# One 256-column operand for the high and low parts of the rows in tiles of 128 rows

## What is computed

```python
def _moe_ref(x, w_gate, w_noise, noise, w1, w2):     # D=192, E=8, F=1024
    ...
    for e in range(E):
        for k in range(2):
            mask = top2[:, k] == e
            ...
            h = np.maximum(x[mask] @ w1[e], 0.0)
            out[mask] += top2_w[mask, k, None] * (h @ w2[e])
def _moe2_ref(x, w_gate, w1, w2):
    ...
        xe = x[mask]
        h = np.maximum(xe @ w1[e], 0.0)
        ye = h @ w2[e]
        out[mask] = gate_w[mask, None] * ye
```

## Time and profile before

| | us |
|---|---|
| median of 3 runs | 1208.05 (1206.38 to 1210.27) |
| the profiled execution | 1204.87 |
| its span, first to last instruction | 1203.1 |
| PE busy | 1090.5 (91%) |
| DVE busy | 793.1 (66%) |
| ACT busy | 591.3 (49%) |
| POOL busy | 526.6 (44%) |

### The profile page before, as it was taken

How to read it: one execution, slowest core, us unless ns; L and a number is a source line. 1 busy time by engine, 2 the same in 40 slices (tenths; PEclk the granted TensorE clock), 3 DMA queues, 4 the chain that set the end, 5 groups by cost and what they waited for, 6 DMA issues and landing times.

```text
span 1203.1 us, 28405 instructions
## 1 busy us (share of the span) xinstructions
PE 1090.5 (91%) x8218; PEld 1053.8 (88%) x8219; DVE 793.1 (66%) x1352; ACT 591.3 (49%) x1082; POOL 526.6 (44%) x621
## 2 busy tenths in 40 slices
PE   3962999999999999999999999999999888999995
PEld 1541989999999999999999999988999888999995
DVE  9998889996787554555595545545655964655652
ACT  2340555665654555667535445445754434444442
POOL 1000456665444544443455544444443434545552
PEclk9985899999999999999999999999998989999998
DMA  7152223324522326421327233266432473543510
GB/s 248 53 164 74 67 63 89 84 80 145 147 87 83 110 76 211 148 88 63 86 78 220 90 89 107 77 201 181 123 103 66 138 215 104 143 121 105 143 42 22
DMA packets 97780, 136.47 MB, mean 113 GB/s; under 512 B 25994, under 2 KB 75981, under 8 KB 97484
## 3 DMA queue, kind: packets, MB, share of 16 engines
q1 hardware_dynamic: 78284, 92.96, 26.0%
q0 software_dynamic: 19456, 43.04, 12.3%
HBM read 104.74 MB, written 34.54 MB: 116 GB/s over the span
## 4 chain that ended last, share of the span: by engine, by line
PE 62%; DVE 17%; issue 8%; DMA 7%; ACT 2%; DVEq 1%; POOL 1%; ACTq 0%; POOLq 0%; SPq 0%; PEldq 0%
PE ps_y L1492 18%; PE ps_y L1493 8%; PE ps_h L1462 6%; PE ps_h L1472 6%; PE ps_h L1466 6%; PE ps_h L1463 6%; PE ps_h L1469 6%; DMA row<-x_rows,read_now 5%; DVE prod L592 4%; DVE h_lo L923 2%; PE ps_x L1448 2%; PE ps_x L1449 1%; DVE prod L604 1%; DVE prod L809 1%; PE ps_route L1396 1%
## 5 line engine op out<-in xcount | busy, mean ns | idle before, releaser
L1492 PE MATMUL ps_y<-w_hl,h_hi 128*128 128x384 f32 x1480 | 451.8, 369 | 15.8 <-DVE h_lo L923 15.2
L923 DVE SCALAR_TENSOR_TENSOR h_lo<-ps_h,h_hi 128x512 fp32r<-128x512 f32 x404 | 258.9, 685 | 241.0 <-ACT h_hi L1238 205.2
L1493 PE MATMUL ps_y<-w_hl,h_lo 128*128 128x192 f32 x1480 | 373.6, 252 | 0.0
L1238 ACT ACTIVATE h_hi<-ps_h 128x512 fp32r<-128x512 f32 x404 | 219.4, 595 | 220.3 <-PE ps_h L1472 209.1
L1492 PEld LDWEIGHTS ps_y<-w_hl,h_hi 128*128 128x128 f32 x1480 | 282.1, 191 | 21.5 <-DVE h_lo L923 20.3
L1493 PEld LDWEIGHTS ps_y<-w_hl,h_lo 128*128 128x128 f32 x1480 | 286.5, 194 | 0.0
L488 POOL DMA_INDIRECT row<-x_rows,read_now x202 | 229.5, 1136 | 119.6 <-POOL read_now L484 81.9
L1462 PE MATMUL ps_h<-xa_hi,w1a_hi 128*128 128x256 f32 (+1 forms) x808 | 234.8, 291 | 8.4 <-issue 5.3
L1466 PE MATMUL ps_h<-xa_lo,w1a_hi 128*128 128x256 f32 (+1 forms) x808 | 230.1, 285 | 2.1 <-DVE xa_lo L912 2.1
L1472 PE MATMUL ps_h<-xb_lo,w1b_hl 128*128 128x256 f32 (+1 forms) x808 | 229.8, 284 | 0.0
L1463 PE MATMUL ps_h<-xa_hi,w1a_lo 128*128 128x256 f32 (+1 forms) x808 | 229.2, 284 | 0.0
(11 more groups left out here) (184 smaller groups left out, 1328.3 us busy)
## 6 DMA issues: line engine op xcount, KB each, us to landing
w_raw<-in_moe_w_dram SPq DMA_DIRECT2D x32, 768.0 KB
w1a_raw<-in_moe_w_dram SPq DMA_DIRECT2D x32, 512.0 KB
w1b_raw<-in_moe_w_dram SPq DMA_DIRECT2D x64, 256.0 KB
x_pad<-in_x_dram SPq DMA_DIRECT2D x2, 2688.0 KB, 10.4
x_pad<-y_rows SPq DMA_DIRECT2D x14, 384.0 KB
prod<-y_rows SPq DMA_DIRECT2D x14, 384.0 KB
x_rows<-tok SPq DMA_DIRECT2D x4, 1344.0 KB
row<-x_rows,read_now POOLq DMA_INDIRECT x202
```

Of the source, the lines that this page charges most:

```text
L923: nc.vector.scalar_tensor_tensor(out=h_lo[:, i * GF:(i + 1) * GF, :], in0=ps_h[:, i, :].rearrange("p (f t) -> p f t", f=GF), scalar=0.0, i ...
L1238: act.activation(h_hi[:, i * GF:(i + 1) * GF, :], ps_h[:, i, :].rearrange("p (f t) -> p f t", f=GF), ACT.Relu).then_inc(h_hi_ready, 1)
L1492: nc.tensor.matmul(ps_y[:, u, 0:2 * D], h_hi[:, i, cols], w2_hl[b][:, f, :], start=(i == 0), stop=False)
L1493: last = nc.tensor.matmul(ps_y[:, u, 0:D], h_lo[:, i, cols], w2_hl[b][:, f, 0:D], start=False, stop=(i == FC - 1))
```

## The change

The high and the low part of a row tile now stand side by side in one buffer (`xa[:, 0]` and `xa[:, 1]`, the same for `xb`). Tiles of 256 rows compute as before. A half tile takes another way on three engines.

- PE (`up_half`): w1a_hi meets the high and low parts in one matmul of 256 columns, w1b_hl the same, and w1a_lo meets xa_hi in 128. The first block has four matmuls, the other seven have three: 25 in place of 40. What belongs to the high parts lands in one half of a block of ps_h, what belongs to the low parts in the other. The groups become ready one by one.
- ACT copies the second halves of a group out of ps_h (`copy_part`, 256 columns). DVE adds the first halves (`sum_parts`, 256 columns). ACT rectifies the sum to h_hi (`high_of_sum`), and DVE makes h_lo of it (`low_of_sum`). ACT's order is copy 0, copy 1, high 0, the side work, copy 2, high 1, copy 3, high 2, high 3; DVE's is its side work, sum 0, sum 1, low 0, sum 2, low 1, sum 3, low 2, low 3.
- ACT and DVE choose the way with a branch in every tile. DVE's registers for the next expert are loaded in `next_expert`, ahead of the groups, instead of behind them.

```diff
-        xa_hi = sb("xa_hi", [P, T], F32R)
-        xa_lo = sb("xa_lo", [P, T], F32R)
-        xb_hh = sb("xb_hh", [P, T], F32R)
-        xb_lo = sb("xb_lo", [P, T], F32R)
+        xa = sb("xa", [P, 2, T], F32R)
+        xb = sb("xb", [P, 2, T], F32R)
+        xa_hi, xa_lo = (xa[:, i, :] for i in range(2))
+        xb_hh, xb_lo = (xb[:, i, :] for i in range(2))
         h_hi = sb("h_hi", [P, FC, T], F32R)
         h_lo = sb("h_lo", [P, FC, T], F32R)
+        sum_more = sb("sum_more", [P, T])
...
+        h_part = tok_T[:, 1, :].rearrange("p (i f t) -> p i f t", i=2, t=P)
+        h_sum = [buf.rearrange("p (f t) -> p f t", t=P) for buf in (tok_T_b[:, 1, :], sum_more[:, :])]
...
+        def half_parts(i):
+
+            return [ps_h[:, i, :].rearrange("p (f v t) -> p v f t", f=GF, v=2)[:, v, :, :] for v in range(2)]
...
+            def next_expert(p, j):
+
+                with dve.If(dve.snap(expert_at) == j):
...
+                    dve.reg_load(expert_at, table[p][0:1, bass.ds(e * 4 + 1, 1)])
+                    dve.reg_load(half_at, table[p][0:1, bass.ds(e * 4 + 2, 1)])
+                    dve.reg_mov(split_1a_at, j)
+                    dve.reg_sub(split_1b_at, expert_at, 1)
...
+            def split_w1_ahead(p, j):
+
+                with dve.If(dve.snap(split_1a_at) == j):
+                    split_w1a(*ahead())
...
+            def sum_parts(g0, j, i):
+
+                dve.wait_ge(h_part_copied, (g0 + j) * NG + (i + 1))
+                if i > 1:
+                    dve.wait_ge(h_lo_ready, (g0 + j) * NG + (i - 1))
+                nc.vector.tensor_tensor(h_sum[i % 2], half_parts(i)[0], h_part[:, i % 2, :, :],
+                                        ALU.add).then_inc(h_summed, 1)
+
+            def low_of_sum(g0, j, i):
+
+                dve.wait_ge(h_hi_ready, (g0 + j) * NG + (i + 1))
+                nc.vector.scalar_tensor_tensor(
+                    out=h_lo[:, i * GF:(i + 1) * GF, 0:P], in0=h_sum[i % 2], scalar=0.0,
+                    in1=h_hi[:, i * GF:(i + 1) * GF, 0:P].bitcast(F32), op0=ALU.max, op1=ALU.subtract).then_inc(h_lo_ready, 1)
...
-                for i in range(NG):
-                    dve.wait_ge(h_hi_ready, (g0 + j) * NG + (i + 1))
-                    nc.vector.scalar_tensor_tensor(
-                        out=h_lo[:, i * GF:(i + 1) * GF, :], in0=ps_h[:, i, :].rearrange("p (f t) -> p f t", f=GF),
-                        scalar=0.0, in1=h_hi[:, i * GF:(i + 1) * GF, :].bitcast(F32), op0=ALU.max, op1=ALU.subtract).then_inc(h_lo_ready, 1)
+                if weights:
+                    next_expert(p, j)
+                with dve.If(dve.snap(half_at) == j):
+                    for i in range(NG):
+                        sum_parts(g0, j, i)
+                        if i > 0:
+                            low_of_sum(g0, j, i - 1)
+                    low_of_sum(g0, j, NG - 1)
+                with dve.Else():
+                    for i in range(NG):
+                        dve.wait_ge(h_hi_ready, (g0 + j) * NG + (i + 1))
+                        nc.vector.scalar_tensor_tensor(
+                            out=h_lo[:, i * GF:(i + 1) * GF, :], in0=ps_h[:, i, :].rearrange("p (f t) -> p f t", f=GF),
+                            scalar=0.0, in1=h_hi[:, i * GF:(i + 1) * GF, :].bitcast(F32), op0=ALU.max, op1=ALU.subtract).then_inc(h_lo_ready, 1)
+                    dve.sem_inc(h_summed, NG)
...
-            def tile(p, g0, n, b0, j, ahead):
-
-                for i in range(NG):
-                    act.wait_ge(h_ps, (g0 + j) * NG + (i + 1))
-                    act.activation(h_hi[:, i * GF:(i + 1) * GF, :], ps_h[:, i, :].rearrange("p (f t) -> p f t", f=GF),
-                                   ACT.Relu).then_inc(h_hi_ready, 1)
-                    if i == NG // 2 - 1:
-                        side_early(p, j)
-                        if ahead is not None:
-                            with act.If(j == b0):
-                                split_w1a(*ahead)
-                        side_late(p, j)
-                        act.sem_inc(ps_x_free, 1)
+            def mid_tile(p, j, b0, ahead):
+
+                side_early(p, j)
+                if ahead is not None:
+                    with act.If(j == b0):
+                        split_w1a(*ahead)
+                side_late(p, j)
+                act.sem_inc(ps_x_free, 1)
+
+            def copy_part(g0, j, i):
+
+                act.wait_ge(h_ps, (g0 + j) * NG + (i + 1))
+                act.activation(h_part[:, i % 2, :, :], half_parts(i)[1], ACT.Copy).then_inc(h_part_copied, 1)
+
+            def high_of_sum(g0, j, i):
+
+                act.wait_ge(h_summed, (g0 + j) * NG + (i + 1))
+                act.activation(h_hi[:, i * GF:(i + 1) * GF, 0:P], h_sum[i % 2], ACT.Relu).then_inc(h_hi_ready, 1)
+
+            def copy_high(g0, j, i):
+
+                act.wait_ge(h_ps, (g0 + j) * NG + (i + 1))
+                act.activation(h_hi[:, i * GF:(i + 1) * GF, :], ps_h[:, i, :].rearrange("p (f t) -> p f t", f=GF),
+                               ACT.Relu).then_inc(h_hi_ready, 1)
+
+            def tile(p, g0, n, b0, full, j, ahead):
+
+                with act.If(j < full):
+                    for i in range(NG // 2):
+                        copy_high(g0, j, i)
+                with act.Else():
+                    for i in range(NG // 2):
+                        copy_part(g0, j, i)
+                    high_of_sum(g0, j, 0)
+                mid_tile(p, j, b0, ahead)
+                with act.If(j < full):
+                    for i in range(NG // 2, NG):
+                        copy_high(g0, j, i)
+                    act.sem_inc(h_part_copied, NG)
+                with act.Else():
+                    for i in range(NG // 2, NG):
+                        copy_part(g0, j, i)
+                        high_of_sum(g0, j, i - 1)
+                    high_of_sum(g0, j, NG - 1)
...
+            def up_half(p, g0, j, b):
+
+                for f in range(FC):
+                    cols = slice(f * P, (f + 1) * P)
+                    at = f % GF * T
+                    dst = ps_h[:, f // GF, at:at + T]
+                    if f == 0:
+                        nc.tensor.matmul(dst[:, 0:P], w1a_hi[b][:, cols], xa[:, 0, 0:P], start=True, stop=False)
+                        nc.tensor.matmul(dst[:, 0:P], w1a_lo[b][:, cols], xa[:, 0, 0:P], start=False, stop=False)
+                        pe.wait_ge(x_lo_ready, 2 * (g0 + j) + 1)
+                        nc.tensor.matmul(dst[:, P:T], w1a_hi[b][:, cols], xa[:, 1, 0:P], start=False, stop=False)
+                        pe.wait_ge(x_hi_ready, 2 * (g0 + j) + 2)
+                        pe.wait_ge(x_lo_ready, 2 * (g0 + j) + 2)
+                    else:
+                        nc.tensor.matmul(dst, w1a_hi[b][:, cols], xa[:, :, 0:P], start=True, stop=False)
+                        nc.tensor.matmul(dst[:, 0:P], w1a_lo[b][:, cols], xa[:, 0, 0:P], start=False, stop=False)
+                    last = nc.tensor.matmul(dst, w1b_hl[b][:, cols], xb[:, :, 0:P], start=False, stop=True)
+                    if f % GF == GF - 1:
+                        last.then_inc(h_ps, 1)
+                    if f == FC // 2 + 1:
+                        side(p, j)
...
+                if rows == T:
+                    up(p, g0, j, b)
+                    order = sorted(range(FC), key=place_of)
+                else:
+                    up_half(p, g0, j, b)
+                    order = range(FC)
```

62 lines of the change are left out of this document (33 added, 29 removed).

## The result

| | us, median | ratio to before | 95% interval |
|---|---|---|---|
| before | 1207.22 (1204.55 to 1210.27, 4 runs) | 1 | |
| changed | 1239.57 (1237.76 to 1247.06, 4 runs) | 1.0279 | 1.0230 to 1.0328 |

The changed kernel is slower by 2.8%, some 34 us. The forecast was 1212, range 1201 to 1221, with 0.45 on a loss clear of noise. The sign of its middle was right and its size far off.

What follows compares the result with a forecast made beforehand. Most tiles were taken to go at PE's pace, some at DVE's. Terms -7.9 + 5.8 + 4.0 + 1.0 + 1 = +3.9 us on the profiled 1204.87 gave 1208.8, or 1212 on the median's scale, range 1201 to 1221.

Steps and rivals of the forecast that it cites:

- What PE saves: Up part of each half tile on PE: 2.94 us in place of 4.44, two-piece operands at the price of one.
- Free half tiles: Five half tiles without side work: a gain of 1.3 us each, bounds 0.8 and 1.5, 6.5 us in all.
- The stall forecast at the low of group 1: Down part of free half tiles: PE stalls 0.2 us because the low of group 1 comes late.
- Tiles that wait for gathered rows: Four half tiles at 420.06, 674.17, 751.47 and 810.90: gain 0, since a shorter up part only waits longer for the gather.
- the sign named for it: Profile sign for the four gather tiles: longer waits for the gathered rows.
- Entangled tiles: Half tiles at 205.05, 248.07, 537.57, 885.61: staging queued behind a high awaiting DVE's late sum; losses 5.8 and 4.0 us per pair.
- the upper bound: Four entangled half tiles: a loss of about 4 us each, should idle time bring the clock down too.
- Tiles with marks: Half tiles at 627.23 and 957.54, DVE late with marks: loss 0.5 us each, 1.0 for both.
- Light side work: Half tiles at 584.35 and 918.88, copies of groups 2 and 3 behind scoring or counting: gains 0.4 and 1.0 us.
- All half tiles: All 17 half tiles, the forecast's gains and losses without the branches: 2.9 us lost.
- Branches: Added branches on ACT and DVE in 101 tiles, table reads moved ahead of groups: 1 us, between 0 and 8.
- slower by code and clock: Rival, chance 0.18: ten tiles miss ACT or DVE instructions by 1 us, entangled tiles lose 4 us of clock; 1224 us.

Runs made afterwards that it cites:

- product_long: Kernel before with PE's shorter up part in half tiles, the product's halves never added, and 14 never-run matmuls per half tile padding PE's code: 0.9872, 1196.2 us.
- stage_first: Changed kernel with ACT's staging and other mid-tile work ahead of the high of group 0 in half tiles, instead of behind it: ratio 1.0214 to the kernel before.
- both_long: Changed kernel with table reads behind the groups, staging ahead of the high of group 0, and 14 never-run matmuls per half tile padding PE's code: 1.0071.

## Why the prediction was right or wrong

- **What PE saves** was right: in four of the five free half tiles the up part takes 2.96 to 3.03 us for 2.94, in the fifth 4.96 for 6.42 before. Two pieces cost the same as one.
- **Free half tiles** were right, 6.6 us in all for 6.5, with some luck: the five gain 2.1, 0.9, 1.4, 0.9 and 1.3 us, where 1.3 each and 0.8 to 1.5 were given. With nobody to add, they gain 10.4. The stall forecast at the low of group 1 is there: the third block of the down part starts 0.49 us after the second (1125.80 to 1126.29), where a block takes 0.29.
- **Tiles that wait for gathered rows**: 0 forecast, +3.0 in the profiled execution. The mechanism is right where the sum is left out: in product_long the four tiles wait 7.3 us for rows, for 3.7 before, and gain nothing (+0.7). In the changed kernel the sign named for it did not come: three of the four don't wait for rows at all, and the fourth 2.6 us. Another wait ends last there, that for the lows. ACT loads a table before its first copy, as it did before its first high in the kernel before (also 1.28 us), and now the chain behind it is longer:

```profile
428.92 1.28 ACT L1290 ACT_TABLE_LOAD   x1 [0.19 <-issue]
430.21 0.66 ACT L1290 ACTIVATE tok_T<-ps_h 128x256 f32<-128x256 f32 x2
431.09 0.42 ACT L1295 ACTIVATE h_hi<-tok_T_b 128x256 fp32r<-128x256 f32 x1 [0.22 <-DVE tok_T_b L936]
432.21 0.39 ACT L1290 ACTIVATE tok_T<-ps_h 128x256 f32<-128x256 f32 x1 [0.70 <-issue]
```

  PE waited 1.5 us for the lows of this tile. How that ends goes with the granted clock: the same tile takes 9.17 us at 0.83 in the changed kernel, and in stage_first 7.72 at 1.00, with 0.9 us of waiting for lows and 0.4 for rows.
- **Entangled tiles**: the step was right and a little small: 12.3 us for 9.8. Missing was the clock, which I had kept for the upper bound. Tile 205.05 lost 3.5 for 2.9, as PE's next 3.3 us went at 0.50. PE's idle time ahead of the turning was 3.93 us, where 2 to 3 were named.
- **Tiles with marks**: 3.2 for 1.0. Undersized, since the clock fell here too: 0.72 over the tile at 627.23, for 0.83.
- **Light side work**: 3.4 us gained for 1.4. This column also moved by -2.8 and +4.4 us where PE's product was untouched, so the difference says little.
- **All half tiles**: 2.9 forecast (the sum without the branches), 8.5 measured.
- **Branches**: this is the step that failed. "Each of 101 tiles gets three more on ACT and two more on DVE, with table reads moved ahead of the groups. ACT and DVE mostly wait there for PE ... I take 1 us, between 0 and 8." Full tiles lost 25.4: 16.8 in the four first tiles of experts, 4.4 in the four where PE's code is at issue, 4.2 in the rest. The cover named was the wait for PE. It is real in most tiles, and gone in those where DVE comes last, which the forecast itself lists elsewhere. I priced branches and reads as one small thing and never asked what the reads stood behind before. They stood behind issued operations (977.59 to 979.99), where the sequencer's time is free. Undone, they give 11 us back, and the branches alone cost 5. The sign named for this, more idle time of DVE ahead of its groups than 34.4 us, failed as well: the changed kernel has 17.6 us of it ahead of the lows of full tiles (L963), in 9 waits, where L923 had 34.4 in 22. It is a few long waits in the wrong tiles that cost, 3.6 us in one, and the sum hides them.
- **The rival "slower by code and clock"**, 1224, had the right direction and put the code on the wrong engines. The misses found are PE's, and they came from code that became shorter. Its sum is off too: ten tiles by 1 us and 4 us of clock are 14 us, not the 12 that it adds.

What remains open: the clock was not tested by itself. In the full tiles of both_long, 12.3 us remain. The branches and the low clock are in them, and no run parts these two. The price of adding the halves, some 19 us, is a difference of three runs.

## What to carry to other kernels

The register loads cost nothing here behind operations that were already issued, and their full time ahead of the first one where the engine came late. So for each moved scalar step, ask what covered it, in the tiles where its engine is last. When a change splits one engine's step into a ping-pong of two engines, everything queued behind the new wait inherits the other engine's lateness: put the work that others wait for ahead of it, or use the change only where there is no side work. And take a change of code length as a change of its own: pad it back before you judge the rest.

## What was not expected of the hardware

- Fewer instructions on PE brought it new standstills. Shortening the code by 30 instructions in each half tile brought gaps of 2.1 to 3.0 us at two places, and padding that is never run took some 10 us off (0.9872 for 0.9963).
- One register load from a table in on-chip memory takes 0.30 to 0.36 us at some places and 0.7 to 1.05 us at some others. Of the long ones on DVE, PE and ACT, 3 of 6 in the kernel before and 6 of 10 in the changed one came while SP issued a store of a block of rows (2.3 to 4.4 us each). That the two are linked was not tested.
- PE did 255 matmuls less and was busy just as long, while the granted clock went from 0.966 to 0.946.
